# A linear-attention, dense and routed-expert kernel on one core: order of the first group's steps, of VectorE's work at the handover, and of the expert loop's loads and halves

## What is computed

```python
# linear attention, B, H, S, D = 4, 8, 768, 48, for every t
cur = einsum('bhd,bhe->bhde', u * k_t, v_t)
y_t = einsum('bhd,bhde->bhe', r_t, state + cur)
state = w * state + einsum('bhd,bhe->bhde', k_t, v_t)
# dense layer, 3072 tokens x 384, hidden 2048
x = max(0.01 * (x @ w_in), x @ w_in) @ w_out
# routed experts, E = 8, hidden 1024, on the rows with x @ w_skip > 0
e = argmax(x @ w_gate); p = softmax(x @ w_gate)[e]
out = x + p * (relu(x @ w1[e]) @ w2[e])     # the other rows: out = x
```

## Time and profile before

| what | value |
|---|---|
| median of 3 executions | 669.46 us (668.72 to 670.49) |
| profiled execution: its own time | 666.72 us |
| profiled execution: span from first to last instruction | 665.0 us |
| granted TensorE clock, mean | 0.996 of full speed |
| TensorE matmuls busy | 646.2 us, 97% of the span |
| VectorE / ScalarE / POOL busy | 401.4 / 309.5 / 86.0 us |
| data moved | 78.09 MB, 117 GB/s on average |

### The profile page before, as it was taken

One profiled execution on the slowest core, in us unless ns is written; L12 is line 12 of the kernel. 1 busy time (PEld: TensorE's weight loads), 2 busy tenths in 40 slices (PEclk: granted clock), 3 DMA queues, 4 the chain that ended last, 5 costly groups with the idle time before them and its releaser, 6 DMA issues.

```text
span 665.0 us, 14201 instructions
## 1 busy us (share of the span) xinstructions
PE 646.2 (97%) x4733; PEld 606.9 (91%) x4734; DVE 401.4 (60%) x867; ACT 309.5 (47%) x683; POOL 86.0 (13%) x102
## 2 busy tenths in 40 slices
PE   8989999999999999999999999999999989999994
PEld 7878999999999999999999999999999879989993
DVE  7876765656656575466555545653466854865752
ACT  5466534345334443454434344333346435746650
POOL 5240000100010001001000100010021141423311
PEclk9999999999999999999999999999999999999998
DMA  8935625220422321242114221201505267686300
GB/s 226 301 130 205 212 72 174 73 71 18 134 68 71 96 75 54 64 143 73 48 30 139 73 72 30 76 8 57 213 1 206 92 199 277 207 284 264 130 21 8
DMA packets 39325, 78.09 MB, mean 117 GB/s; under 512 B 9032, under 2 KB 27494, under 8 KB 39216
## 3 DMA queue, kind: packets, MB, share of 16 engines
q1 hardware_dynamic: 34272, 62.96, 30.2%
q10 hardware_dynamic: 2432, 9.76, 4.3%
q0 software_dynamic: 2560, 4.58, 2.2%
HBM read 61.68 MB, written 13.00 MB: 112 GB/s over the span
## 4 chain that ended last, share of the span: by engine, by line
PE 89%; DVE 3%; ACT 2%; issue 2%; DMA 1%; POOL 1%; SPq 0%; ACTq 0%; POOLq 0%; DVEq 0%
PE bank L808 31%; PE bank L831 30%; PE bank L908 8%; PE bank L925 7%; PE bank L673 3%; PE bank L735 3%; PE bank L742 2%; PE bank L756 1%; PE bank L916 1%; DMA stage<-in_rk_t 1%; PE bank L865 1%; PE bank L901 1%; ACT am L1100 1%; PE bank L716 0%; DMA zg<-z_rows,get 0%
## 5 line engine op out<-in xcount | busy, mean ns | idle before, releaser
L1138 ACT ACTIVATE h_sb<-bank 128x384 f32<-128x384 f32 x128 | 62.8, 491 | 221.6 <-PE bank L808 221.4
L1448 DVE TENSOR_TENSOR h_sb<-h_sb,bank 128x384 f32<-128x384 f32 x128 | 70.9, 554 | 156.2 <-ACT h_sb L1138 156.2
L808 PE MATMUL bank<-x_hi,win_hi 128*128 128x384 f32 x384 | 135.1, 352 | 1.0 <-DVE win_lo L1494 0.6
L831 PE MATMUL bank<-wout_hi,g_hi 128*128 128x394 f32 x384 | 132.0, 344 | 0.4 <-DVE state L1424 0.4
L831 PE MATMUL bank<-wout_hi,g_lo 128*128 128x394 f32 x384 | 131.2, 342 | 0.0
L831 PE MATMUL bank<-wout_lo,g_hi 128*128 128x394 f32 x384 | 131.1, 342 | 0.0
L808 PE MATMUL bank<-x_hi,win_lo 128*128 128x384 f32 x384 | 129.5, 337 | 0.0
L808 PE MATMUL bank<-x_lo,win_hi 128*128 128x384 f32 x384 | 129.3, 337 | 0.0
L1455 DVE TENSOR_TENSOR g_lo<-h_sb,g_hi 128x384 fp32r<-128x384 f32 x128 | 71.8, 561 | 30.7 <-ACT g_hi L1145 29.7
L1145 ACT ACTIVATE g_hi<-h_sb 128x384 fp32r<-128x384 f32 x128 | 66.7, 521 | 42.3 <-DVE h_sb L1448 40.9
L1927 POOL DMA_INDIRECT id_list<-idgate,dst x24 | 24.4, 1016 | 449.0 <-DVE dst L1655 444.1
(11 more groups left out here) (250 smaller groups left out, 895.5 us busy)
## 6 DMA issues: line engine op xcount, KB each, us to landing
raw<-in_experts SPq DMA_DIRECT2D x32, 768.0 KB, 6.0
rkt<-in_rk_t SPq DMA_DIRECT2D x46, 192.0 KB, 3.7
rkn<-in_rk_nat SPq DMA_DIRECT2D x21, 384.0 KB, 4.4
v<-in_v_nat SPq DMA_DIRECT2D x24, 192.0 KB, 3.0
z_rows<-z_sb SPq DMA_DIRECT2D x24, 192.0 KB, 2.8
out<-z_sb SPq DMA_DIRECT2D x24, 192.0 KB, 2.8
stage<-in_win ACTq DMA_DIRECT2D x4, 768.0 KB, 4.5
stage<-in_wout_t ACTq DMA_DIRECT2D x4, 768.0 KB, 6.6
```

The costliest lines, as they stand in the source:

```text
L808: mm = pe.matmul(h_ps[t % 2][:, 0:GT], a[:, kk, cols], b[G % 2][:, kk, :], start=n == 0, stop=n == 3 * KT - 1)
L831: mm = pe.matmul(z_ps[i][:, 0:ZW], a[t % 3][:, tok], b[:, f, :], start=f == 0 and j == 0, stop=f == FT - 1 and j == 2)
L1138: act.activation(h_sb[t % 2][:], h_ps[t % 2][:, 0:GT], ACT.Copy, scale=SLOPE).then_inc(s_h_scaled, 1)
L1448: dve.tensor_tensor(h_sb[t % 2][:], h_sb[t % 2][:], h_ps[t % 2][:, 0:GT], ALU.max).then_inc(s_leaky, 1)
```

## The change

In the first group ScalarE's diagonal of chunk 3 comes ahead of the load of the next `wout`, VectorE updates the states ahead of the first low part, and the routing tables are made in step 13. `gates_turned` comes behind `project`. At the handover the three pieces of expert 0's `w2_lo` are made at other places, `id_get` is made inside the chain that makes the plan, and block 0's rows are turned into two banks with a copy for the first third by itself, behind two more matmul pairs of the early block. In the expert loop relu reports each half, the first product finishes its first half earlier, TensorE loads the next block's entries before the second half product, two pieces of w2 come before relu and one behind, and SP loads w1 of the next expert ahead of w2. The diff, cut:

```diff
@@ sync, expert loads
-            def report(e):
-                sp.wait_ge(raw1_load[e % 2], 32 * (e // 2 + 2))
-                sp.sem_inc(s_w1_in, 1)
-                sp.wait_ge(raw2_load[e % 2], 32 * (e // 2))
-                sp.sem_inc(s_w2_in, 1)
...
-            for e in range(AHEAD, E):
...
-                load_w1(e)
...
-                load_w2(e, raw2, raw2_load)
-                report(e)
+            next_w1(AHEAD)
+            report_w1(AHEAD)
+            for e in range(AHEAD, E):
+                if e + 1 < E:
+                    next_w1(e + 1)
+                next_w2(e)
+                if e + 1 < E:
+                    report_w1(e + 1)
+                report_w2(e)
@@ tensor
             def second_product_a(i, parts):
                 pe.wait_ge(s_eht_a_lo, 2 * i + parts[-1] // 4 + 1)
-                pe.wait_ge(s_w2_lo, PIECES)
+                pe.wait_ge(s_w2_lo, -(-DM * (parts[-1] + 1) // PIECE))
...
+            def turn_first_rows():
+                pe.wait_ge(s_eht_a_hi, 2)
+                pe.wait_ge(s_eht_a_lo, 2)
+                pe.transpose(zt_0_ps[:, 0:P], zg[0][:, 0:P], ident).then_inc(s_zt_0_done, 1)
+                for kk in range(1, KT):
+                    mm = pe.transpose(zt_ps[:, P * kk:P * kk + P], zg[0][:, P * kk:P * kk + P], ident)
+                mm.then_inc(s_zt_done, 1)
...
+            def first_product(par, base, first=False):
+                terms = (zt_hi, w1_hi), (zt_hi, w1_lo), (zt_lo, w1_hi)
                 for kk in range(KT):
+                    if kk == 1 and first:
+                        pe.wait_ge(s_zt_lo, 1)
+                    for (a, b), c in (itertools.product(terms, range(2)) if kk < KT - 1 else
+                                      ((t, c) for c in range(2) for t in terms)):
...
+                        if kk == KT - 1 and a is zt_lo:
+                            mm.then_inc(s_eh_done, 1)
+            def turn_hidden(j):
                 for f in range(EFT):
+                    if f % 4 == 0:
+                        pe.wait_ge(s_relu_done, 2 * j + f // 4 + 1)
...
-                if step in (3, 7, 11):
-                    gates_turned((step + 1) // 4)
                 if step + AHEAD >= STEPS:
                     turn_rows_a(step + AHEAD - STEPS)
                 project(step)
+                if step in (3, 7, 11):
+                    gates_turned((step + 1) // 4)
...
             blocks = pe.value_load(...)
+            load_entries(pe, regs, 0)
+            second_product_a(1, range(4, 6))
             pe.wait_ge(rows_in[0], 16)
-            turn_rows(0)
-            second_product_a(1, range(4, 6))
+            turn_first_rows()
+            second_product_a(1, range(6, 8))
             pe.wait_ge(s_w1_lo, PIECES)
-            pe.wait_ge(s_zt_lo, 1)
-            first_product(0, 0)
-            second_product_a(1, range(6, 8))
+            pe.wait_ge(s_zt_0_lo, 1)
+            first_product(0, 0, True)
             pe.wait_ge(rows_in[1], 16)
             turn_rows(1)
-            pe.wait_ge(s_relu_done, 1)
-            turn_hidden()
+            turn_hidden(0)
...
-                            cur, odd, _, _, nxt, nxt_odd = entries(pe, regs, j)
+                            cur, odd, _, _, nxt, nxt_odd = loaded_entries(pe, regs)
...
                             with pe.If(j < blocks - 1):
-                                pe.wait_ge(s_relu_done, j + 2)
-                                turn_hidden()
+                                turn_hidden(j + 1)
+                            load_entries(pe, regs, j + 1)
                             second_product(u % 2, odd * EW, 1)
@@ scalar
                 if step == 0:
+                    set_diag(3, range(H))
                     load_stage(5)
-                    set_diag(3, range(H))
...
+            def turned_first_rows():
+                act.wait_ge(s_zt_0_done, 1)
+                act.activation(zt_hi[0][:, 0, :], zt_0_ps[:, 0:P], ACT.Copy).then_inc(s_zt_0_hi, 1)
+                act.wait_ge(s_zt_done, 1)
+                act.activation(zt_hi[0][:, 1:, :]..., bank[4][:, P:DM], ACT.Copy).then_inc(s_zt_hi, 1)
+            def hidden_rows(j):
+                for half in range(2):
+                    act.wait_ge(s_eh_done, 2 * j + half + 1)
+                    act.activation(eh[:, 512 * half:...], bank[half][:], ACT.Relu).then_inc(s_relu_done, 1)
...
-                                high_w2(1 - odd, range(1))
+                                high_w2(1 - odd, range(2))
...
-                                high_w2(1 - odd, range(1, PIECES))
+                                high_w2(1 - odd, range(2, PIECES))
@@ vector
             chained(dve.tensor_copy(w_state[:], ...))
-            dve.wait_ge(s_const2_in, 16)
-            dve.memset(cum[:, 0, :], 0.0)
-            dve.tensor_scalar(off[:], ...)
-            dve.tensor_scalar(edges[:], ...)
-            linked(dve.tensor_copy(idgate[:, :, 0]..., ...))
             leaky(1)
-            low_out_first(slice(0, 1))
             for n in range(CPG):
                 update_state(n)
+            low_out_first(slice(0, 1))
             low_g(1)
...
+                if step == FT - 3:
+                    routing_tables()
+                if step == STEPS - 3:
+                    low_w2_early(0, (0,))
                 if step + 2 < STEPS:
                     low_g(step + 2)
...
-                if step + AHEAD >= STEPS:
-                    low_w2_early(0, (step + AHEAD - STEPS,))
             copy_logits()
             route_a(GROUPS - 1)
-            low_w2_early(0, (2,))
             route_gates(GROUPS - 1)
             take_ranks(GROUPS - 1)
             route_spots(GROUPS - 1)
+            low_w2_early(0, (1,))
...
             turned_hidden_a(0)
+            low_w2_early(0, (2,))
...
             linked(dve.tensor_reduce(eidf[:], cmp[:], AX.X, ALU.add))
+            dve.wait_ge(s_found, 16)
+            dve.tensor_scalar(id_get[:], found[:, :, 0], ...).then_inc(s_spots, 1)
...
-            dve.wait_ge(s_found, 16)
-            dve.tensor_scalar(id_get[:], found[:, :, 0], ...).then_inc(s_spots, 1)
             turned_hidden_a(1)
...
-                                low_w2(e, odd, range(1))
+                                low_w2(e, odd, range(2))
...
-                                low_w2(e, odd, range(1, PIECES))
+                                low_w2(e, odd, range(2, PIECES))
```

90 lines of the change are left out of this document (53 added, 37 removed).

## The result

The changed kernel took 662.11 us (median of 4 executions, 661.89 to 662.72), the kernel before 669.09 in the same comparison (4 executions, 668.60 to 670.49): a ratio of 0.990, 95% interval 0.988 to 0.992. I had forecast 664.1 and a range of 662.2 to 667.0; the median of the four lies 0.1 under the range, three of the four lie under it, and "faster" had 0.86.

What follows compares the result with a forecast made beforehand. TensorE, full from 49 to 513 us, bounds the kernel; only 7.3 us of idle time elsewhere can go. 2.7 + 1.5 + 0.3 + 0.9 = 5.4 us takes 666.72 to 661.3, plus 2.74 gives 664.1, range 662.2 to 667.0.

Steps and rivals of the forecast that it cites:

- First group: 26 to 49 us: waits for states 0.43, masked scores 1.56, win_lo 0.44 and gates 0.25 go, 2.7 us in all.
- The tables: First group, VectorE: routing tables leave the path for step 13, so leaky(1) starts 1.2 us earlier.
- The diagonal: First group, ScalarE: scalings start at 31.4 instead of 33.75, and TensorE's 1.56 us wait for masked scores goes.
- of 0.57, 0.13 stays: First group: of TensorE's 0.57 us wait for win_lo, 0.13 remains.
- rival (2): First group gives half back, mask, win_lo and wout_lo following each other on busy engines: 1.35 kept, 665.4 us; chance 0.12.
- The turned gates: First group: turned gates go behind project(3), and the 0.25 us wait for the gates' copy goes.
- Handover: Dense layers to experts: earlier logits, list and gather, register load out of the path, less a new stall: gain 1.5 us.
- the new stall: Handover, first matmul of the second early block: TensorE waits 1.1 us for VectorE's low half.
- Loop: Expert loop, jump back: register load ahead of the second half product is covered, gaining 0.3 us; SP's order gives nothing.
- Rival (4): Expert loop: relu over 1.3 us late in every block exposes the load and branches 12 times, 676.0 us; chance 0.04.
- End: Last block: one w2 piece ahead of relu removes the 0.96 us eht_lo wait, less some 0.1 for the load: 0.9.
- The offset: 2.74 us, by which the median of the runs shown lies above the profiled execution, added to reach 664.1.

Runs made afterwards that it cites:

- two_more: Changed kernel plus second early block's first low half right behind id_get, TensorE's plan wait and loads later, win_lo ahead of g_lo: 661.06 us.
- half_first: Changed kernel plus VectorE making the second early block's first low half right behind id_get, ahead of the rest of the plan's chain: 662.38 us.
- diag_back: Changed kernel with ScalarE's load of the next wout again ahead of chunk 3's diagonal: 663.66 us.
- before_sp_order: Kernel before with only SP's order of the experts' loads and reports changed: 666.82 us, ratio 0.998.

## Why the prediction was right, and where not

**The bound.** Right in the main: in the long middle TensorE is idle for 0.09 us before and for none after, and all of the gain but the gates of steps 7 and 11 lies in the three places. But those gates gave 0.5 us out of the stretch that the table of windows calls full: a wait of 0.37 on the weight side shows there as under 0.1 of idle time. And of the 1.86 us behind 546, 0.9 was only the end of TensorE's work at 656.1, and so not to be had.

**First group, forecast 2.7.** Measured 1.5 between the first profile and the changed one, 0.95 against the second profile of before, and with the gates of steps 7 and 11, another 0.5 to 0.6. (The six profiles that have the changed first group as it is need 33.93 to 34.39 to `hidden(8)`.) Step by step:
- *The tables "leave the path ... 1.2".* Failed. The 1.00 us row for 128 x 24 numbers was not work: it ended at 28.79, 0.03 behind GpSimd's product (27.72 + 1.04), and in the thirteen other profiles it is 0.17 long, in three of them at the same place in the program. Taken out, it left the wait to the next such row. Measured worth 0 to 0.4.
- *The diagonal "starts when ScalarE is free, 31.4".* Failed with it. The sum for diag needs GpSimd's ruk, ready at 31.4 in the changed profile, and g_lo ahead of it was lengthened by the same product to 31.84; so diag came at 32.3. The mechanism was right (the load of the next wout held the scalings), its size is 0.6 to 1.5 for 1.56.
- *win_lo, "of 0.57, 0.13 stays".* Failed: 1.15 stayed in that profile, 0.7 to 1.1 in others. I went straight from win_hi to win_lo and left out g_lo, which stands between mask and win_lo in VectorE's order. At 0.55 it would have cost little by my own times; but the mask ended at 36.27, 0.6 later than forecast (35.25, and 0.4 for the later `hidden(0)`), and g_lo took 1.15. two_more took it out of the way, and 0.5 stayed, with win_lo waiting for win_hi. My rival (2), half of the first group given back, came near to what happened, though by this and not by full engines.
- *"The turned gates ... the 0.25 goes."* Right in kind, counted once: the diff has three steps, and undoing it costs 0.8.

**Handover, forecast 1.5.** Measured 1.64, from 30.02 to 28.38 between the last projection and block 1. The logits are read 0.5 earlier, the new stall is 0.97 for 1.1 and at the matmul I named, the gathered rows are not waited for, relu and zt_lo end the last wait at 0.53. The register load "stood in this path, and the change takes it out": 1.23 when put back, for 0.86; its row was 1.09 long there, and another 0.72 passed between its end and the product. I also wrote that this trace does not contradict the 600 ns that the Trainium skill (DMA: Bandwidth & Descriptors, Latency and other measured facts) gives as a floor. It does: TensorE's load of the block count at line 991 took 0.487 us in it. Piece 0's new place is step 125 and lies between leaky(127) and g_lo(127); the forecast's 45 and 47 are wrong numbers for them, and nothing hangs on that. That undoing single parts costs 1.23, 1.06 and 0.35, more than 1.64 together, is no contradiction: the stall of 0.97 is the price paid for id_get's place, and half_first and two_more get it back.

**Loop, forecast 0.3.** The number came, 0.34 to 0.48, but not for the reason that I gave. I credited the load on TensorE's queue and put SP's order at "off TensorE's path, nothing". With the load put back the gap stayed away, and with SP's order alone on the kernel before it went, so SP's order is enough by itself. SP's report of w1 made ScalarE late, relu ended at 580.8, TensorE's sequencer passed it only then and lost its lead, and the load that came next was short of cover. I had read the idle row's end and not what had delayed the sequencer 3 us earlier. Whether the load's new place alone, with SP's old order, would close the gap too was not run; that my step was idle is shown only beside SP's new order. Rival (4) did not occur: no block waits for relu.

**End, forecast 0.9.** Measured 0.92, with 0.7 shown to be the second piece's place. The 0.1 that I took off for the load inside the last block is not there: with the load back at its old place the stretch is the same 13.51. And the last us behind it did not "stay as they are": 9.05 for 8.87.

**The offset.** The sum was made against 666.72 and then 2.74 was added, the distance to the median of three. That put the profile's share of luck into the forecast: those three were probably of the lower clock (their clock is not on record), the changed kernel's four mostly not. From 667.13, the like-clock median, 5.4 less gives 661.7; measured were 662.1.

**Open.** The state updates ahead of the first low part, the split copies of block 0's rows and relu by halves were not undone one by one, so no run shows what each is worth. The last 0.1 between `hidden(8)` and the last projection; the diagonal's size between 0.6 and 1.5; and the first group's own spread, 35.34, 35.87 and 37.14 us in three profiles that have this part in common.

## What to carry to other kernels

A row far longer than its shape's others may hold a wait, though no idle time stands before it: look what ran beside it before its time goes into a sum, because taking the instruction out hands the wait to the next one. A gap without a releaser behind a register load is to be followed back through that engine's sequencer to the last semaphore it passed, and from there to the queue that set it. And a median should be moved by a difference of profiles only when the profile's own place among the executions is known, here by the granted clock.

## What the runs showed of the hardware

**VectorE and GpSimd shut each other out, and the later one pays.** g_lo at 30.48 takes 1.36 beside GpSimd's product of 30.21 to 31.42: it ends 0.42 behind it, and alone it takes 0.55. wout_lo at 32.23 behind kn (31.39 to 32.73) takes 1.71; in the first profile of the kernel before it takes 1.34, and GpSimd's next product, which started 0.22 behind it at 32.16, takes 2.01 for 1.02 instead. Rows that read PSUM (leaky, the mask) and the one-input reduction keep their 0.54 to 0.56 and 1.38. The Trainium skill (SBUF — State Buffer, SBUF: two separate sides) says that the two share a port pair as an exclusive lock held for the whole instruction, which a VectorE operation takes when it is in a two-port mode, or has two SBUF inputs while GpSimd's operation reads SBUF. By that rule the 0.83 us above edges' own 0.17 were never work; the trace agrees, with 28.79 against 28.76 for the two ends. No trace shows that edges, which has one input, was in such a mode.

**TensorE's clock can fall early in the program.** In 7 of the 14 profiles (those with a mean clock of 0.995 or more) the stretch to `hidden(0)` ran at a granted clock of 1.00 throughout. In the other 7 it fell, at 12.8 to 15.4 us. In diag_back, by the table of windows:

```profile
12.00:14.00 2.00, 1.74 (x36) 1.52 (x34) 2.00 (x4) 1.67 (x7) 1.69 (x3) 0.98 1.21 355
14.00:16.00 2.00, 2.00 (x42) 2.00 (x40) 1.67 (x4) 0.97 (x4) 0.59 (x3) 0.50 0.97 379
16.00:18.00 2.00, 2.00 (x22) 1.88 (x18) 0.40 (x1) 0.49 (x1) 0.00 (x0) 0.50 1.04 263
18.00:20.00 2.00, 2.00 (x11) 1.19 (x7) 1.69 (x3) 0.00 (x0) 0.00 (x0) 0.50 1.01 266
```

That is the lower level, 1.2 GHz for 2.4, and TensorE had stood idle for 0.9 of the 2.0 us from 10 to 12. `hidden(0)` then started at 24.93, against 21.77 to 22.45 in most profiles at full clock: 1 to 3 us that no part of the change touches. The two classes of executions of the kernel before lie 2.5 us apart, where lowest and highest are 4.7 apart. The clock is not the whole of the early spread: in before_sp_order the clock stayed at 1.00 and `hidden(0)` still came at 23.61, behind 1.8 us of waits for GpSimd's am. Nor does the idle time by itself say when the clock falls: in that run TensorE stood idle for 1.33 of the 2.0 us from 10 to 12 and kept its clock, in two_more for 0.32, and it fell. What decides it is open.
